# Taking the low part of an inner activation one slot later, in an attention and two-MLP kernel

## The reference

```
q_rot, k_rot = rotate(q), rotate(k)              # 2 x 8 heads, 576 tokens, head size 64, float32
attn = softmax(q_rot @ k_rot^T / 8)
x = (attn @ v), heads side by side               # 1152 tokens x 512
h = x @ w_in;   x = (h * sigmoid(h)) @ w_out     # 512 -> 2048 -> 512, "layer 0"
h = x @ w_in2;  out = elu(h) @ w_out2            # 512 -> 2048 -> 512, "layer 1"
```

## Time and profile before

| | before |
|---|---|
| runs, us | 582.81, 584.43, 584.81 (median 584.43) |
| the profiled execution: its time | 583.76 |
| its span, first to last instruction | 582.0 |
| granted TensorE clock, mean | 0.994 |
| PE busy | 540.8 us, 93% |
| DVE busy | 296.1 us, 51% |
| ACT busy | 350.9 us, 60% |
| POOL busy | 346.9 us, 60% |
| chain of work that ended last | PE 73%, DVE 13%, ACT 6%, issue 3% |

### The profile page before, as it was taken

One profiled execution on the slowest core, in us unless ns is written; L12 is line 12 of the kernel. 1 busy time (PEld: TensorE's weight loads), 2 busy tenths in 40 slices (PEclk: granted clock), 3 DMA queues, 4 the chain that ended last, 5 costly groups with the idle time before them and its releaser, 6 DMA issues.

```text
span 582.0 us, 9268 instructions
## 1 busy us (share of the span) xinstructions
PE 540.8 (93%) x3308; PEld 530.0 (91%) x3308; DVE 296.1 (51%) x505; ACT 350.9 (60%) x726; POOL 346.9 (60%) x284
## 2 busy tenths in 40 slices
PE   1577789999999999999999999999999999999998
PEld 1476679999999999999999999889999999999997
DVE  4659966663237785325664434877244550047500
ACT  2667868776557666546786555766555773356531
POOL 3857787967764654654664564444544666656662
PEclk9979999999999999999999999999999999999999
DMA  6666562645544535434435333323443444334450
GB/s 239 184 170 177 165 205 74 172 114 178 164 120 137 136 90 159 139 108 144 133 93 156 110 97 124 110 74 112 123 117 105 133 123 134 125 119 128 117 162 29
DMA packets 43229, 77.16 MB, mean 133 GB/s; under 512 B 5296, under 2 KB 12848, under 8 KB 43184
## 3 DMA queue, kind: packets, MB, share of 16 engines
q1 hardware_dynamic: 41456, 74.21, 43.6%
q10 hardware_dynamic: 1728, 2.36, 1.1%
HBM read 63.57 MB, written 2.36 MB: 113 GB/s over the span
## 4 chain that ended last, share of the span: by engine, by line
PE 73%; DVE 13%; ACT 6%; issue 3%; DMA 2%; POOL 1%; SPq 0%; ACTq 0%; DVEq 0%; POOLq 0%
PE banks L899 59%; PE banks L864 4%; PE banks L836 3%; PE banks L822 3%; PE banks L824 2%; DVE neg_max L611 2%; DVE banks L685 2%; DVE act_buf L683 2%; DMA k_st<-k_raw 1%; ACT act_buf L487 1%; ACT g_hi L494 1%; ACT prob L435 1%; PE banks L843 1%; DVE pt_lo L618 1%; DVE g_lo L691 1%
## 5 line engine op out<-in xcount | busy, mean ns | idle before, releaser
L321 POOL TENSOR_TENSOR w_lo<-w_raw,w_hi 128x512 fp32r<-128x512 f32 x192 | 247.7, 1293 | 203.7 <-ACT w_hi L475 203.1
L475 ACT CAST w_hi<-w_raw 128x512 fp32r<-128x512 f32 x189 | 116.9, 621 | 43.6 <-PE banks L899 39.7
L899 PE MATMUL banks<-x_lo,w_hi 128*128 128x384 f32 x384 | 130.1, 339 | 0.2 <-DVE x_lo L651 0.2
L899 PE MATMUL banks<-g_lo,w_hi 128*128 128x384 f32 x384 | 129.0, 336 | 0.0
L899 PE MATMUL banks<-x_hi,w_lo 128*128 128x384 f32 x384 | 128.6, 335 | 0.0
L899 PE MATMUL banks<-g_hi,w_lo 128*128 128x384 f32 x384 | 128.5, 335 | 0.0
L899 PE MATMUL banks<-x_hi,w_hi 128*128 128x384 f32 x384 | 128.4, 334 | 0.0
L899 PE MATMUL banks<-g_hi,w_hi 128*128 128x384 f32 x384 | 128.4, 334 | 0.0
L611 DVE TENSOR_REDUCE neg_max<-banks 128x1 f32<-128x576 f32 x72 | 54.3, 754 | 66.3 <-PE banks L824 65.2
L822 PE MATMUL banks<-k_st,q_one 128*128 128x288 f32 x160 | 53.0, 346 | 32.0 <-DVE q_two L665 13.6
L435 ACT ACTIVATE prob<-banks,neg_max 128x576 f32<-128x576 f32 x72 | 53.6, 744 | 39.0 <-DVE neg_max L611 38.4
(11 more groups left out here) (74 smaller groups left out, 721.7 us busy)
## 6 DMA issues: line engine op xcount, KB each, us to landing
w_raw<-w SPq DMA_DIRECT2D x192, 256.0 KB, 2.6
q_raw<-q SPq DMA_DIRECT2D x11, 384.0 KB, 3.0
q_one<-q_raw SPq DMA_DIRECT2D x44, 96.0 KB, 2.6
k_raw<-k SPq DMA_DIRECT2D x7, 576.0 KB, 4.3
k_st<-k_raw SPq DMA_DIRECT2D x28, 144.0 KB, 2.6
v_raw<-v SPq DMA_DIRECT2D x8, 320.0 KB, 3.0
out<-act_buf ACTq DMA_DIRECT2D x12, 192.0 KB, 2.7
q_two<-q_raw SPq DMA_DIRECT2D x22, 96.0 KB, 2.4
```

The lines of the kernel that those rows point to most:

```text
L321: nc.gpsimd.tensor_tensor(w_st[LO][:, slot, :], w_raw[:, slot, :], w_st[HI][:, slot, :].bitcast(F32), ALU.subtract).then_inc(w_lo_done, 1)
L475: nc.scalar.copy(w_st[HI][:, slot, :], w_raw[:, slot, :]).then_inc(w_hi_done, 1)
L899: last = nc.tensor.matmul(dst, w_st[wp][:, slot, m * P:(m + 1) * P], src[xp][:, tile, :], start=start and n == 0, stop=stop and n == 2)
```

## The change

On ScalarE, `hidden_hi` is called for unit n - 2 and not n - 1, and stands right behind `hidden_act(n - 1)`. On VectorE, `hidden_mul` is split: `hidden_first` (L679, or L683 in layer 1) and `hidden_second` (L685, layer 1 alone). The slot's order becomes `hidden_first(n - 1)`, `max_tile` (tiles 0 and up), `hidden_lo(n - 2)`, `hidden_second(n - 1)` or `layer_lo(n - 1)`, and then the rest; for tile -1 `probs_lo` moves behind them. On TensorE, `spread_sums` moves from j = 5 to j = 6. No instruction is added or taken away, and no wait changes its target.

More of the change, by code:

```diff
@@ L699, in layer_lo @@
                                         x[c % 2][HI][:, dt, :].bitcast(F32), ALU.subtract).then_inc(y_lo_done, 1)
-            def evict_a(n):
+            def evict_first(n):
                 if n >= 0 and n % 32 < FT:
[L703 to L710, removed]
+                    hidden_first(n)
[7 more added lines that the diff above has]
+                    hidden_lo(n)
             for par in range(2):
```

## The result

The changed kernel took 575.42, 575.45, 575.65 and 576.10 us, median 575.55 (forecast 577.7, range 575.9 to 581.0); ratio to the kernel before 0.9857, 95% interval 0.9838 to 0.9876. The profiled execution took 576.10 us, span 574.3. Timed again on another occasion, the same kernel took 577.71 us (median of six), ratio 0.9906 (0.9887 to 0.9926).

What follows compares the result with a forecast made beforehand. PE was taken to bound the kernel, waiting for VectorE beside layer 1; -7.16 + 0.52 + 0.26 = -6.38 us gave 577.4 from the profiled 583.76, 578.05 from the median, middle 577.7 us, range 575.9 to 581.0.

Steps and rivals of the forecast that it cites:

- The mechanism: Hidden units of layer 1: VectorE stands still 0.56 us per unit awaiting ScalarE's high part; a later low part removes PE's waits.
- Layer 1, the gain: PE waits beside layer 1's hidden units go: 2.68, 3.78 and 0.70 us in the three chunks, together 7.16 us.
- The openings: First units of a chunk wait for late low parts: net +0.52 us in the first chunk, +0.26 third, nothing second.
- the wait for `probs_lo`: First chunk's opening, PE's wait at 96.15: covered in the new order, giving back 0.62 us.
- The sum: Whole kernel: -7.16 + 0.52 + 0.26 = -6.38 us on the profiled execution's 583.76.
- The steady bank ring: Plain hidden units: activation, first operation, low part, then bank of unit n + 1; 1.98 us against 2.08, 0.10 to spare.
- The first rival: Bank ring longer than 2.08 us, every plain hidden unit pays the excess; 588.0 us with slower VectorE operations; chance 0.05.
- The other rivals: Ring 0.05 us too long, 579.6 (0.12); ScalarE takes over in layer 1, 580.9 (0.15); moved `spread_sums` costs its saving, 579.4 (0.05).
- VectorE's pace: VectorE's hidden-unit evictions: an independent operation starts 0.47 us behind one lasting 0.56; a full 0.56 would leave 0.01 spare.
- `spread_sums`: Moved one slot later, its 1.7 us of waits go, already inside layer 1's sum; no further gain or cost taken.

Runs made afterwards that it cites:

- late_high: Changed kernel with the high part of unit n - 2 behind the weights in ScalarE's slot; 506.49 us from unit 0, 591.86 us in one run.

## Why the prediction was right or wrong

It was wrong in that the time, 575.55, lies 0.35 us below the range. The mechanism was right; the size of one term was not, and it had nothing to do with the change.

- *Layer 1, the gain.* Right. 2.68, 3.78 and 0.70 us were written, 2.70, 3.79 and 0.76 measured (the third from unit 4 of chunk 3 to the end, 125.39 against 124.63).
- *The openings.* Right in place and sign: 0.66 and 0.48 us at units 3 and 4 were 0.64 and 0.34, the wait for `probs_lo` went and gave back 0.55 us where I had 0.62; net 0.44 for 0.52. Third chunk 0.23 for 0.26.
- *The sum.* -6.38 us written, -6.55 measured by the profiles from unit 0.
- *The steady bank ring.* 0.10 us to spare, 0.09 measured. The first rival did not come. Its price per unit was wrong: in the third chunk late_high paid the excess once in two units, half as much as I had counted, but beside attention it paid 9.3 us in two chunks where ten units at 0.34 make 3.4.
- *The other rivals* did not come either: the stretches beside layer 1 are at their floor and PE waits there for nobody, so ScalarE did not take over and the moved `spread_sums` costs nothing.
- *VectorE's pace.* 0.47 us between operations that don't depend on each other held in the new order too (522.07 to 522.54 to 523.01, each 0.55 or 0.56 long). That goes against the first lines of the section "The DRAIN you can't avoid" of the Trainium skill's page "VectorE: DVE Perf Modes", and agrees with what it says further on of an operation that is not held.
- *A small misreading.* `end_lo` in the earlier trace rows ends at 223.90 + 0.56 = 224.46, so `value_products` start 0.10 us behind it, not 0.07; nothing in the sum rests on it.
- *`spread_sums`.* Nothing taken, nothing measured on top of the low part. That the three transposes went without a wait is right, that the move did it is not: the low part alone does.
- *The step that failed* is the last one, from the sum to a time and its lower end: "the full gain with no opening cost and a quick execution (583.76 - 7.2 = 576.6, less 0.7)". The prediction gives no source for the 0.7; the three runs that it had went down to 582.81, 0.95 below the profiled 583.76. What the 0.7 had to cover is the part ahead of the loop. In all 17 profiles an execution is the start of unit 0, the time from unit 0 and another 5.0 us; unit 0 began at 80.02 us in the profile that I counted from, and anywhere from 78.05 to 82.91 in the eight profiles of the two kernels, so 2.0 us quicker was possible. With the change's 6.55 us alone that execution would take 577.21; the profiled one of the changed kernel took 576.10, and the 1.11 between them is unit 0 at 78.91. The median of 575.55 lies 1.66 below 577.21, which puts unit 0 near 78.4 (an estimate from these sums). The four runs that the change was first judged by were quick ones (575.4 to 576.1, all with a mean granted clock of 0.994; of eight later ones of the same kernel none was below 576.67, and six had 0.985 to 0.988). Why those four lie together is not shown. Of the 8.6 us between the medians 6.55 are the change's, the other 2 are not.

## What to carry to other kernels

Where two engines hand a tile to and fro inside a slot, the one that waits for its own result loses the other's time in every turn (0.56 us here), and does so though it is half idle. Taking that step one slot later, between operations on the next tile, made the loss vanish, as long as the path to the freed buffer stayed inside the slack. In the slots without attention that path could be added up from start-to-start distances to 0.01 us; beside attention my count of who is covered did not hold. Do it only in the stage that needs it: here layer 1 gained 7.25 us and layer 0 lost 0.7. Compare two kernels from a mark behind the noisy part; two medians that differ by 1.4% held 0.3% of luck in the part that both have in common.

## What was not expected

The time until unit 0 begins varied from 78.05 to 82.91 us over eight profiles of two kernels with the same code there, while the 2304 matmuls behind it, with all waits, repeated within 0.13 us. The moment at which one copy lands moved by 3.2 us of it; a lower granted clock afterwards (0.81 or 0.85 against 0.93 over 46 us) went with another 1.2 to 2.8 us. And where no attention stood beside the units, a shortage in a ring over three banks and two evicting engines cost PE once in two units: 4.40 us for two units where one path was 0.23 us too long, not twice that.
